# A token mixer of 4 batches on one core: queries and keys of a chunk made by VectorE together

## The reference

```python
mag = np.sqrt(a_re * a_re + a_im * a_im)
scale = np.minimum(mag, 0.999) / (mag + 1e-06)
a_re_n, a_im_n = (a_re * scale, a_im * scale)
for t in range(S):
    ar, ai = (a_re_n[:, :, t, :, None], a_im_n[:, :, t, :, None])
    new_re = ar * S_re - ai * S_im
    new_im = ar * S_im + ai * S_re
    kv = np.einsum('bhd,bhe->bhde', k[:, :, t], v[:, :, t])
    S_re, S_im = (new_re + kv, new_im)
    y[:, :, t] = np.einsum('bhd,bhde->bhe', q[:, :, t], S_re)
...
h = xt @ U @ V
u = x + h.transpose(0, 2, 1)
ch = np.maximum(u @ w_ch1, 0.0) @ w_ch2
...
theta = x @ w_theta
zr, zi = x * np.cos(theta), x * np.sin(theta)
y = np.einsum('ts,bsd->btd', w_tok_r, zr) + np.einsum('ts,bsd->btd', w_tok_i, zi)
u = x + y
return (u + np.maximum(u @ w_ch, 0.0)).astype(np.float32)
```

## Time and profile before

| what | value |
|---|---|
| median of three runs | 926.39 us (925.23 to 927.0) |
| the profiled execution | 924.23 us, its span 922.5 us |
| TensorE matmul busy | 823.2 us, 89% of the span |
| VectorE busy | 501.2 us, 54%, 844 instructions |
| ScalarE busy | 389.9 us, 42% |
| GpSimd busy | 268.3 us, 29%, 249 instructions |
| L867 and L875 (queries) | 24 and 48 instructions of 384 columns, mean 588 and 1203 ns |
| L513 and L516 (keys) | 24 and 48 instructions of 384 columns, mean 1313 and 1229 ns |
| mean granted TensorE clock | 0.982 of full |

### The profile page before, as it was taken

The page is one execution under the profiler, slowest core; times in us unless marked ns, Lnnn a source line. Parts: engine busy times, 40 slices in busy tenths (PEclk is TensorE's granted clock), DMA queues, the critical chain, the costliest instruction groups (busy, mean ns, idle before and its releaser), DMA issues.

```text
span 922.5 us, 14046 instructions
## 1 busy us (share of the span) xinstructions
PE 823.2 (89%) x5424; PEld 750.2 (81%) x5424; DVE 501.2 (54%) x844; ACT 389.9 (42%) x783; POOL 268.3 (29%) x249
## 2 busy tenths in 40 slices
PE   0157989799999898999999998999999898999998
PEld 0016769699998777998999786998999786999998
DVE  6775528854645644955544653955644652121544
ACT  4474735554333553643322552653323453121321
POOL 5386537552201442420101452430000341020100
PEclk9977999899999999999999999999999999999999
DMA  9041124536553111021064121003054113000062
GB/s 305 2 141 35 57 81 144 180 123 213 217 175 129 53 61 52 18 79 59 23 222 137 50 85 53 18 4 134 1 211 156 61 53 137 2 1 1 35 214 77
DMA packets 43505, 87.61 MB, mean 95 GB/s; under 512 B 6480, under 2 KB 36432, under 8 KB 43440
## 3 DMA queue, kind: packets, MB, share of 16 engines
q1 hardware_dynamic: 43440, 86.72, 28.0%
HBM read 72.55 MB, written 14.16 MB: 94 GB/s over the span
## 4 chain that ended last, share of the span: by engine, by line
PE 75%; DVE 13%; issue 4%; ACT 3%; DMA 2%; POOL 2%; SPq 0%; DVEq 0%; POOLq 0%
PE bank L1082 69%; PE bank L1113 2%; PE bank L1119 1%; DVE region L883 1%; DVE qk L875 1%; DMA out<-out_sb 1%; PE bank L1182 1%; PE bank L1263 1%; PE bank L1196 1%; DVE hT L978 1%; DMA stream<-in_w_tok 1%; ACT region L611 1%; DVE x_sb L988 1%; DVE qf L867 1%; DVE phasor L815 1%
## 5 line engine op out<-in xcount | busy, mean ns | idle before, releaser
L1082 PE MATMUL bank<-uT,w_sb 128*128 128x384 f32 x864 | 172.6, 348 | 4.6 <-DVE uT L972 4.6
L1082 PE MATMUL bank<-hT,w_sb 128*128 128x384 f32 x864 | 165.9, 338 | 1.9 <-DVE hT L978 1.9
L1082 PEld LDWEIGHTS bank<-uT,w_sb 128*128 128x128 f32 x864 | 154.0, 192 | 10.5 <-issue 5.7
L1082 PE MATMUL bank<-tok,z 128*128 128x384 f32 x864 | 159.0, 338 | 0.0
L1082 PEld LDWEIGHTS bank<-hT,w_sb 128*128 128x128 f32 x864 | 151.8, 189 | 4.0 <-DVE hT L978 4.0
L1082 PEld LDWEIGHTS bank<-tok,z 128*128 128x128 f32 x864 | 149.5, 188 | 0.8
L513 POOL TENSOR_TENSOR kf<-stream,shrink 128x384 f32<-128x384 f32 x24 | 31.5, 1313 | 219.1 <-PE bank L1082 125.8
L665 ACT ACTIVATE hT<-bank 128x384 fp32r<-128x384 f32 x96 | 46.5, 484 | 101.7 <-PE bank L1082 101.7
L978 DVE SCALAR_TENSOR_TENSOR hT<-bank,hT 128x384 fp32r<-128x384 f32 x96 | 52.9, 553 | 62.9 <-ACT hT L665 62.8
L505 POOL TENSOR_TENSOR xs<-x_sb,xs 128x384 fp32r<-128x384 f32 x24 | 25.6, 1079 | 155.5 <-ACT xs L680 155.5
L1082 PE MATMUL bank<-region 96*128 96x128 f32 x384 | 53.5, 283 | 10.5 <-DVE region L883 8.8
(11 more groups left out here) (208 smaller groups left out, 1406.3 us busy)
## 6 DMA issues: line engine op xcount, KB each, us to landing
tok<-w_tok_split SPq DMA_DIRECT2D x48, 768.0 KB, 4.4
w_tok_split<-tok_part SPq DMA_DIRECT2D x24, 384.0 KB, 3.1
stream<-in_q SPq DMA_DIRECT2D x24, 192.0 KB, 2.4
stream<-in_k SPq DMA_DIRECT2D x24, 192.0 KB, 2.6
stream<-in_v SPq DMA_DIRECT2D x24, 192.0 KB, 3.4
stream<-in_w_tok SPq DMA_DIRECT2D x24, 192.0 KB, 3.1
out<-out_sb SPq DMA_DIRECT2D x24, 192.0 KB, 1.9
stream<-in_a_re SPq DMA_DIRECT2D x19, 192.0 KB, 3.2
```

Of the source, the lines that this page charges most:

```text
L1082: return t.matmul(o, lhsT, rhs, start=start, stop=stop, is_transpose=turned)
```

## The change

The two scale factors and the two scaled operands now lie side by side (`scales`, `scaled`), as q and k do in their buffer. VectorE makes queries and keys in three instructions of 768 columns: one multiply by the scales, then one by cosine and one by sine, which are read twice with a step of zero. The output is a pair of blocks of `qk`: the queries and that of the two key buffers which the chunk uses. GpSimd makes no keys, and its weight pieces follow one another. VectorE takes over GpSimd's waits; the semaphores for keys are gone, and everybody who waited for them waits for the queries' one alone.

```diff
-        grow, shrink = sb("grow", [P, D]), sb("shrink", [P, D])
-        qf, kf = sb("qf", [P, D]), sb("kf", [P, D])
+        scales = sb("scales", [P, 2, D])
+        grow, shrink = scales[:, 0, :], scales[:, 1, :]
+        scaled = sb("scaled", [P, 2, D])
+        qf, kf = scaled[:, 0, :], scaled[:, 1, :]
...
             def load_qkv_behind(b, c):
                 sp.wait_ge(s_Q.sem, s_Q.at(b, c - 2))
-                sp.wait_ge(s_K.sem, s_K.at(b, c - 2))
...
             def batch(b, last):
                 b_next = b + 1
-                for c in range(1, C):
-                    if c >= 2:
-                        pool.wait_ge(s_kt.sem, s_kt.at(b, 2 * (c - 1)))
-                        pool.wait_ge(s_kv.sem, s_kv.at(b, c - 1))
-                    keys(b, c)
-                    if b == 0 and 2 <= c < 2 + KD:
-                        split(2 * PIECES + c - 2)
+                if b == 0:
+                    for n in range(2 * PIECES, STAGED):
+                        split(n)
...
-                if not last:
-                    keys(b_next, 0)
-
             quotients(0, True)
             for n in range(2 * PIECES):
-                if n == 2 * PIECES - 2:
-                    keys(0, 0)
                 split(n)
...
             def queries(b, c):
                 dve.wait_ge(s_qkv_in[c % 3].sem, s_qkv_in[c % 3].at(b, c // 3 + 1))
                 dve.wait_ge(s_exp.sem, s_exp.at(b, c + 1))
-                d.tensor_tensor(qf[:, :], qkv[:, c % 3, 0, :], grow[:, :], ALU.mult).then_inc(s_qf.sem, 1)
-                dve.wait_ge(s_qf.sem, s_qf.at(b, c + 1))
                 if c >= 1:
                     dve.wait_ge(s_qt.sem, s_qt.at(b, 2 * c))
                 elif b:
                     dve.wait_ge(s_ch.sem, s_ch.at(b - 1, KD))
+                if c >= 2:
+                    dve.wait_ge(s_kt.sem, s_kt.at(b, 2 * (c - 1)))
+                    dve.wait_ge(s_kv.sem, s_kv.at(b, c - 1))
+                d.tensor_tensor(scaled[:, :, :], qkv[:, c % 3, 0:2, :], scales[:, :, :], ALU.mult).then_inc(s_qf.sem, 1)
+                dve.wait_ge(s_qf.sem, s_qf.at(b, c + 1))
                 dve.wait_ge(s_phasor.sem, s_phasor.at(b, C))
+                pair = qk[:, :].rearrange("p (i h r d) -> p i h r d", i=3, h=H, r=2)[:, 0:2 + c % 2:1 + c % 2]
                 for j in range(2):
-                    ins = d.tensor_tensor(Qn[:, :, j, :], qf[:, :].rearrange("p (h d) -> p h d", h=H),
-                                          phasor[:, c, j, :].rearrange("p (h d) -> p h d", h=H), ALU.mult)
+                    turned = phasor[:, c, j, :].rearrange("p (h d) -> p h d", h=H)
+                    ins = d.tensor_tensor(pair[:, :, :, j, :], scaled[:, :, :].rearrange("p i (h d) -> p i h d", h=H),
+                                          turned.unsqueeze(1).broadcast_to([P, 2, H, HD]), ALU.mult)
                 ins.then_inc(s_Q.sem, 1)
```

More of the change, by code:

```diff
@@ L189, in token_mixer_program @@
         s_Q = sem("s_Q", C)
-        s_kf = sem("s_kf", C)
-        s_K = sem("s_K", C)
         s_qt = sem("s_qt", 2 * C)
@@ L506, in x2_rest @@
                     .then_inc(s_x2_lo.sem, 1)
-            def keys(b, c):
-                pool.wait_ge(s_qkv_in[c % 3].sem, s_qkv_in[c % 3].at(b, c // 3 + 1))
-                pool.wait_ge(s_exp.sem, s_exp.at(b, c + 1))
-                if b and c == 0:
-                    pool.wait_ge(s_ch.sem, s_ch.at(b - 1, KD))
-                g.tensor_tensor(kf[:, :], qkv[:, c % 3, 1, :], shrink[:, :], ALU.mult).then_inc(s_kf.sem, 1)
-                pool.wait_ge(s_kf.sem, s_kf.at(b, c + 1))
-                for j in range(2):
-                    ins = g.tensor_tensor(Kn[:, c % 2, :, j, :], kf[:, :].rearrange("p (h d) -> p h d", h=H),
-                                          phasor[:, c, j, :].rearrange("p (h d) -> p h d", h=H), ALU.mult)
-                ins.then_inc(s_K.sem, 1)
             def batch(b, last):
                 b_next = b + 1
-                for c in range(1, C):
-                    if c >= 2:
-                        pool.wait_ge(s_kt.sem, s_kt.at(b, 2 * (c - 1)))
-                        pool.wait_ge(s_kv.sem, s_kv.at(b, c - 1))
-                    keys(b, c)
-                    if b == 0 and 2 <= c < 2 + KD:
-                        split(2 * PIECES + c - 2)
+                if b == 0:
+                    for n in range(2 * PIECES, STAGED):
+                        split(n)
                 if not last:
@@ L604, in decays @@
                     act.wait_ge(s_Q.sem, s_Q.at(b, c))
-                    act.wait_ge(s_K.sem, s_K.at(b, c))
-                a.activation(grow[:, :], bank[7][:, 0:D], ACT.Exp)
-                a.activation(shrink[:, :], bank[7][:, 0:D], ACT.Exp, scale=-1.0).then_inc(s_exp.sem, 1)
+                a.activation(grow, bank[7][:, 0:D], ACT.Exp)
+                a.activation(shrink, bank[7][:, 0:D], ACT.Exp, scale=-1.0).then_inc(s_exp.sem, 1)
             def to_sbuf_q(b, c, i):
@@ L1114, in transposes @@
                 ins.then_inc(s_qt.sem, 1)
-                pe.wait_ge(s_K.sem, s_K.at(b, c + 1))
                 if 2 * c + i >= 1:
```

## The result

| | before | after |
|---|---|---|
| median of 9 runs each, same chip | 925.05 us (923.12 to 927.0) | 935.78 us (928.58 to 938.42) |
| ratio | 1 | 1.010, interval 1.008 to 1.012 |
| profiled execution | 924.23 us, span 922.5 | 935.87 us, span 934.0 |
| mean granted TensorE clock of it | 0.982 | 0.971 |

The account below looks back on a forecast made before the run. TensorE carries 75% of the chain, so VectorE and GpSimd edits count only where it stands still for them. Terms 2.9 + 2.9 - 1.9 - 0.9 - 0.3 = +2.7 us gave 929.0 us, range 925.2 to 931.5.

Parts of the forecast that it names:

- What bounds the kernel, the three places of a stage: Queries are on the path in chunk 0; in chunk 1 and chunks 2 to 4 the state multiply waits for ScalarE's gains.
- Price of a wide instruction: A VectorE instruction of 768 columns takes 0.95 us with GpSimd idle, three in a row 2.82 us.
- A: Start of batch 0: wide instructions take turns with GpSimd's last two weight pieces, +2.9 us, bounds -0.3 to +3.3.
- B: Boundaries to batches 1, 2 and 3: keys now lengthen VectorE's part to 2.82 us each, +2.9 us in all.
- C: Queries of chunk 1, four times: shorter, without GpSimd's keys beside the state multiply, so the mask starts earlier; -1.9 us.
- D: Chunk 1, four times: the state multiply takes 0.56 instead of 0.78 us, -0.9 us.
- E: Chunk 4: GpSimd's squares of the next batch end before the last state multiply, -0.3 us.
- F: ScalarE's growth and decay, SyncE's loads and the moved or dropped waits: no effect, since all are met early.
- 1: Rival: in batch 0 the weight pieces don't come between the wide instructions; sum -0.5, 925.9 us, chance 0.13.
- 2: Rival: the state multiply really waits for state_sum, so chunks 1 to 4 gain too; sum -1.6, 924.8 us, chance 0.08.
- 3: Rival: wide instructions overlap more, three take 2.6 us; sum +0.9, 927.3 us, chance 0.10.
- 4: Rival: longer TensorE idle time at a boundary lowers its clock, 1.56 us per fall; +4.3, 930.7 us, chance 0.14.

Follow-up runs that it names:

- e4: The changed kernel run again, unedited, in a later set on another chip: 931.93 us, ratio 1.0072 to before.
- e5: The changed kernel with one redundant wait put back into TensorE's transposes (48 instructions of its list): 928.07 us, ratio 1.0031 to before.
- e11: The changed kernel run a third time, unedited, in a later set: 932.13 us, ratio 1.0047 to before.
- e2: The changed kernel with GpSimd's last two of the first twelve weight pieces held behind batch 0's first queries: 928.87 us, ratio 1.0027 to before.
- e6: The changed kernel with a redundant wait put back into SyncE's load_qkv_behind, 12 in all: 933.48 us in a single run.

## Why the prediction was right and wrong

**What bounds the kernel, the three places of a stage**: right. The mask moved by -0.5 in chunk 0 and by -0.24 in chunk 1, and the multiply stayed 0.09 us behind the gains.

**Price of a wide instruction**: right, 0.95 to 0.96 measured where GpSimd was idle, three in 2.81 (0.95 and 2.82 forecast). The 0.86 of the Trainium skill's page "VectorE: DVE Perf Modes" (section on the TRN2 errata) came out low for these too.

**A**: right, +2.87 by the profile, against +2.9; the 3.1 of the kernel with the pieces held agrees but has a part of the clock in it. The queries ended at 77.02 and not near 75.4, because they started 1.7 us late. The upper bound of +3.3 comes out as about +3.1 from the terms named for it. The turns at 71.77 and 72.06 are those that the text drew; by the rule of the page "SBUF — State Buffer" of the Trainium skill (section "Who interferes with whom") the piece that was ready first would go first, and the trace agrees: the piece at 71.77 came ahead of the wide one of 72.06, and each of the two wide ones behind pieces needed 2.5 us.

**B**: right for the instructions, +2.86 against +2.9, but not for TensorE's holes: 0.90, 2.13 and 2.39 us where 1.2, 0.5 and 1.2 were named as the sign. **C** -2.0 against -1.9, **D** -1.0 against -0.9.

**E**: wrong in sign in this profile, and small. The squares come earlier, as the text said, but in batch 1 the first two lie on the last queries and the other two on the state multiply of chunk 4, which takes 1.13 where it took 0.67 or less:

```profile
338.89 0.82 POOL L458 TENSOR_TENSOR tB<-stream 128x384 f32<-128x384 f32 x1
...
343.42 1.13 DVE L881 TENSOR_TENSOR state<-state_sum,gain 128x384 f32<-128x384 f32 x1 [0.57 <-DVE state_sum L876]
```

In the profiles of e4, e5 and e11 TensorE comes out of the same place 0.1 us earlier, as was forecast.

**F is the step that failed.** It put what the change does to SyncE and to the waits at nothing, by looking only at when the waits are fulfilled. They are indeed fulfilled early. But the waits that were taken out were instructions of TensorE's list, and 48 fewer of them moved the instruction fetches of two boundaries onto the loads that SyncE issues ahead of the stores. The stores went out later and landed later still, the third output with them, and the queries stand behind it: +1.5 and +0.95 us in the profile against before, 2.5 to 4 us in TensorE's holes against the kernel with the redundant waits, 3 by the medians, in which a part comes through the clock (0.9772 against 0.9745). That alone lifts the 929.0 to 931 to 933, which is where the two later sets of the changed kernel lie (931.93 and 932.13), in part by luck, since their profiles have stretches at half clock of their own. The text had noted that the queries stand behind a store's wait of 3.42 us, and did not ask what that wait itself hangs on.

**The clock is the second term that was missing.** The sum has no term for it, and the upper end of the range, 931.5, allows for one fall of 1.56 us. The profiled execution paid +4.7 us net in stretches at half clock, and 1.7 more through the late start of batch 0: together over half of the 11.5 us between the two profiled spans.

**Rivals.** 1, 2 and 3 are refuted: the pieces do come between, the multiply follows the gains and the distance between the masks of later chunks is unchanged but for the squares, and a wide one costs its full price. 4 came true at one boundary and at its price: behind the hole of 2.13 us the clock was at half from 512.5 to 515.9, which cost 1.6 us. Of the thirteen profiles only three show a fall in chunk 0 behind a boundary, all of the changed kernel with its late stores (after, e4, e11), but e2 and e6 have holes as long and none, so that the hole brings the fall is likely and not shown. The larger part lay elsewhere: 4.5 us behind the attention of batch 3, a place that the rival didn't name. Over the nine runs the span goes from 926.8 us at a mean clock of 0.980 to 936.7 at 0.969, so what separates the forecast from this set's median is for the most part this. At 0.980 the changed kernel took 926.2 to 927.0 (three runs) and before 922.7 to 924.3 (24 runs, mean 923.5), that is about +3: less than the 2.7 of the arithmetic and the 2.1 or more of the stores together. At the lower clock of 0.976 the same count gives +3.7.

**Open.** How the loss divides between the late stores and the clock over many runs, since the two counts just given don't close; why the first set lost 4 to 5 us more than the later ones of the same kernel; and what decides where the clock falls. The queries of batch 0 start near 71.1 us in seven of the eleven profiles with wide queries, and in all seven the clock was at half from about 52 to 65 us; in the other four it was back by 60.8 or 63.5, and the queries start at 68.9 to 69.3. TensorE's work up to there is the same in all, so this part is probably chance and not the change.

## What to carry to other kernels

Work that stands behind a wait for a DMA inherits everything that makes that DMA late: put it under the wait, ahead of the instruction that waits, and it can cost nothing, as the queries did here (-7 us, a part of it through the clock). Work taken from an idle engine and given to another that is half idle is paid for at the few places where the second is exposed, so price those places and not the busy shares. And when an edit changes the number of instructions of any engine, even waits alone, look again at the times of the DMA issues; putting the same number of redundant waits back is a cheap test of whether the edit's work or its length costs the time.

## What the runs showed of the hardware that wasn't expected

- Behind the first 40 us of the thirteen traces, 38 of 39 DMA issues on SyncE that took over 1 us (1.04 to 2.09, instead of mostly 0.43) had a fetch of 16,384 bytes of instructions begin between 0.66 us ahead of them and 0.21 us behind their start, while 48 others near such a fetch stayed under 1 us; a fetch is 0.9 to 1.8 us long in the DMA records. It was seen in before too (a load of a token weight, 1.19 us at 162.70, with a fetch 0.25 us ahead of it), where nothing hung on it.
- Two wide VectorE instructions beside two GpSimd instructions of 768 columns took 4.96 us, against 1.83 alone, and the GpSimd ones 4.43 against 3.66: turns, at a loss of 3.1 us to one and 0.8 to the other.
- The mean granted clock of one program's nine executions on one chip lay between 0.969 and 0.980, and the spans 10 us apart with it (936.7 and 926.8 us), though every execution had the same instructions.
